# Attention steps of the next batch at other places in TensorE's order, first batch of four

## The reference

```python
# attention with decay: q, k, v, alpha are (4, 8, 768, 48)
for t in range(S):
    state = alpha[:, :, t, :, None] * state + einsum('bhd,bhe->bhde', k[:, :, t], v[:, :, t])
    y[:, :, t] = einsum('bhd,bhde->bhe', q[:, :, t], state)
x = y as (batch, seq, heads * head_dim)              # (4, 768, 384)
# first MLP: U (768, 32), V (32, 768), w_ch1 (384, 1536), w_ch2 (1536, 384)
h = x.transpose(0, 2, 1) @ U @ V
u = x + h.transpose(0, 2, 1)
x = u + maximum(u @ w_ch1, 0) @ w_ch2
# second MLP: w_in (384, 1024), w_spatial (768, 768), w_out (512, 384)
h = maximum(x @ w_in, 0); u, v = the two halves of h
v = (v - mean(v)) / sqrt(var(v) + 1e-6)
out = (u * (einsum('ts,bsd->btd', w_spatial, v) + b_spatial)) @ w_out
```

## Time and profile before

| | |
|---|---|
| median of 3 runs | 728.5 us (727.13 to 729.15) |
| the profiled execution | 727.21 us |
| its span, first to last instruction | 725.0 us |
| mean granted TensorE clock | 0.988 |
| TensorE busy | 696.3 us, 11336 matmuls |
| VectorE, ScalarE, GpSimd busy | 392.6, 340.2, 212.0 us |

### The profile page before, as it was taken

One profiled execution on the slowest core, in us unless ns is written; L12 is line 12 of the kernel. 1 busy time (PEld: TensorE's weight loads), 2 busy tenths in 40 slices (PEclk: granted clock), 3 DMA queues, 4 the chain that ended last, 5 costly groups with the idle time before them and its releaser, 6 DMA issues.

```text
span 725.0 us, 25711 instructions
## 1 busy us (share of the span) xinstructions
PE 696.3 (96%) x11336; PEld 660.6 (91%) x11336; DVE 392.6 (54%) x666; ACT 340.2 (47%) x575; POOL 212.0 (29%) x143
## 2 busy tenths in 40 slices
PE   2689999999999999999999999999999999999998
PEld 2688989899899999999999999999998998999998
DVE  6888665545654654655453415125834852871671
ACT  5887654554654454556444332335532432532422
POOL 6704660410450320351220330461360060043022
PEclk9879999999999999999999999999999999999999
DMA  9415410410401221401100341011110101101001
GB/s 360 169 47 168 163 42 8 154 47 10 149 3 46 80 79 46 156 3 47 37 3 3 101 151 66 33 38 62 65 45 23 66 23 43 65 0 65 0 0 65
DMA packets 16524, 49.48 MB, mean 68 GB/s; under 512 B 1616, under 2 KB 9552, under 8 KB 15920
## 3 DMA queue, kind: packets, MB, share of 16 engines
q1 hardware_dynamic: 16432, 48.09, 18.8%
HBM read 38.65 MB, written 9.44 MB: 66 GB/s over the span
## 4 chain that ended last, share of the span: by engine, by line
PE 92%; ACT 3%; DVE 2%; issue 1%; DMA 1%; SPq 0%; DVEq 0%; ACTq 0%
PE HB L906 25%; PE ZB L994 7%; PE ZB L996 7%; PE ZB L995 7%; PE SB L906 6%; PE SB L782 5%; PE SB L1031 5%; PE ZB L906 4%; PE SB L888 2%; PE SB L1035 2%; PE ZB L1031 2%; PE ZB L1044 2%; PE SB L897 2%; PE SB L843 2%; PE SB L1044 2%
## 5 line engine op out<-in xcount | busy, mean ns | idle before, releaser
L1556 DVE SCALAR_TENSOR_TENSOR hid_lo<-HB,hid_hi 128x384 fp32r<-128x384 f32 x92 | 51.2, 556 | 139.7 <-ACT hid_hi L1238 139.3
L1238 ACT ACTIVATE hid_hi<-HB 128x384 fp32r<-128x384 f32 x92 | 45.3, 492 | 158.6 <-PE HB L906 158.5
L994 PE MATMUL ZB<-hid_hi,w2h 128*128 128x384 f32 x288 | 98.2, 341 | 0.0
L906 PE MATMUL HB<-uh,w1h 128*128 128x384 f32 x276 | 97.8, 354 | 0.2 <-DVE ul L1552 0.2
L996 PE MATMUL ZB<-hid_lo,w2h 128*128 128x384 f32 x288 | 96.5, 335 | 0.0
L995 PE MATMUL ZB<-hid_hi,w2l 128*128 128x384 f32 x288 | 96.3, 334 | 0.0
L906 PE MATMUL HB<-ul,w1h 128*128 128x384 f32 x276 | 92.5, 335 | 0.0
L906 PE MATMUL HB<-uh,w1l 128*128 128x384 f32 x276 | 92.4, 335 | 0.1
L1085 ACT COPY Qd<-Q 48x768 f32<-48x768 f32 x84 | 73.1, 871 | 12.8 <-POOL Q L674 4.3
L731 POOL TENSOR_TENSOR gl<-gf,gh 128x384 fp32r<-128x384 f32 x32 | 33.5, 1048 | 144.1 <-ACT gh L1278 143.8
L674 POOL TENSOR_TENSOR Q<-Q,bk 112x768 f32<-112x768 f32 x14 | 25.6, 1827 | 162.7 <-ACT Qd L1085 162.7
(11 more groups left out here) (269 smaller groups left out, 1516.5 us busy)
## 6 DMA issues: line engine op xcount, KB each, us to landing
Q<-in_q SPq DMA_DIRECT2D x8, 768.0 KB, 6.1
AL<-in_al SPq DMA_DIRECT2D x7, 768.0 KB, 4.5
K<-in_k SPq DMA_DIRECT2D x7, 768.0 KB, 4.2
Vt<-in_v SPq DMA_DIRECT2D x8, 576.0 KB, 3.6
mid<-x2s SPq DMA_DIRECT2D x8, 576.0 KB, 3.7
x<-mid SPq DMA_DIRECT2D x4, 1152.0 KB, 5.4
out<-o_sb SPq DMA_DIRECT2D x24, 192.0 KB, 1.8
x2s<-in_w SPq DMA_DIRECT2D x9, 384.0 KB, 5.1
```

Source lines behind the costliest of these rows:

```text
L906: last = nc.tensor.matmul(dst, weights(x, w), moving(y, m), start=(n == 0 and x == y == 0), stop=(n == total - 1 and y == 1))
L994: nc.tensor.matmul(bank, w2h[:, i, cols], hi, start=(i == 0), stop=False)
L1238: nc.scalar.activation(hid_hi[:, i % HID, :], up_bank(i)[:, 0:TILE], ACT.Relu).then_inc(h_hi, 1)
L1556: nc.vector.scalar_tensor_tensor(hid_lo[:, i % HID, :], up_bank(i)[:, 0:TILE], 0.0, hid_hi[:, i % HID, :].bitcast(F32), ALU.max, ALU.subtr ...
```

## The change

For the first batch the places of the attention steps are no longer worked out by step_slots but written down, one unit index per step, group 0 and then group 1. The other batches keep step_slots.

```diff
 LEAD = [0.07] + [0.0] * (BATCH - 2)
-SLOTS = [step_slots(lead) for lead in LEAD]
+FIRST_SLOTS = [(8, 10, 12, 14, 16, 18, 20, 22, 24, 26, 26, 28, 28, 29), (31, 33, 35, 37, 39, 41, 43, 45, 47, 49, 49, 50, 50, 51)]
+SLOTS = [[[(g, n) for g in range(GROUPS) for n in range(STEPS) if FIRST_SLOTS[g][n] == j] for j in range(len(UNITS1))]]
+SLOTS += [step_slots(lead) for lead in LEAD[1:]]
```

## The result

| | before | after |
|---|---|---|
| median of 22 runs each | 726.93 us (724.74 to 730.2) | 725.49 us (723.81 to 727.42) |
| profiled execution, its span | 727.21, 725.0 | 724.95, 722.8 |

The ratio of the times is 0.9975, with a 95% interval of 0.9965 to 0.9985: by it 1.8 us were gained, between 1.1 and 2.5 (the two medians lie 1.44 apart). The forecast was a gain of 2.3 us, to 726.2.

What follows compares the result with a forecast made beforehand. TensorE was taken to bound the kernel, with holes in the first stretch to save. Gains of 1.5 + 0.77 = 2.3 us off a median of 728.5 gave 726.2 us, 0.32% faster; range 724.3 to 728.3.

Steps and rivals of the forecast that it cites:

- What bounds the kernel: Whole kernel: TensorE is 92% of the chain that ended last; the change moves only entries, so holes count.
- Level 5 and level 6: First stretch, group 0: level 5 behind h6, due 90.44; level 6 starts within 0.1 of 94.79, with h7 already done.
- The term "1.5": Group 0, ahead of level 6: one unit of 1.56 gained less 0.1, so 1.5 us, bounds 1.45 to 1.63.
- The term "0.77": Group 1, ahead of level 3: 2.43 in which h15 stood becomes 1.66, so 0.77 us gained.
- T to KV: Group 0: two units between instead of three; key copies hidden by 0.45, so 0, up to 0.5 us lost.
- AV and Y: Group 0: 0.13 should leave the AV pair and come to Y: 0, bounds 0.13 us either way.
- Levels 7 and T: Group 0: two holes of some 0.2 each stay: 0, bounds 0.45 us gained and 0.85 lost.
- Rival 3: Group 0: KV waits for ScalarE's key copies, 0.5 to 1.4 late; gain 1.8 to 0.9, 727.2 us; chance 0.11.
- Group 1: First stretch: level 3 goes behind h15, two units behind level 2, so the chain of 3.4 fits into 4.28; 0.77 gained.
- rival 1: VectorE let in earlier in group 0, between level 5's sums or before one at 6/7; 725.6 to 726.1; chance 0.13.
- Rivals 2 and 4: Group 0, levels 6 and 7: VectorE waits one more sum, 727.9, chance 0.14; or a whole GpSimd block, 730.0, chance 0.05.

Runs made afterwards that it cites:

- the run with group 0 alone: Against the changed kernel, group 1's steps got their old places back, so only group 0 has new ones; first stretch 115.12 us, profiled execution 724.77 us.

## Why the prediction was right, point by point

**What bounds the kernel.** Right. Nearly all of the gain lies in holes of TensorE in the first stretch. The other two stretches together take 226.6 to 227.0 before, and 227.0, 226.8 and 228.0 after.

**Level 5 and level 6.** The places came out as worked out: level 5 due at 90.44, measured 90.39; level 6 due at 94.72 or 0.15 late, measured 94.68, and 0.08 and 0.03 late in the next two profiles (the last against its own 4.31 per level). Both bounds for VectorE occurred: let in between the sums in the first profile (1.36), behind both in the other two (2.2), where the prediction had taken the second. The request came 2.02 behind the start of level 5 in every profile with the new place, not 1.68; it still fell into the first sum, so nothing hung on it. The cause was shown, not only argued: with the sums moved away the hole went in the old order of steps as well.

**What was mis-sized.** Three terms were, and they partly make up for each other, so it is partly luck that the sum of 2.3 came close to the 2.2 of the profiles.

The term "1.5" rests on a hole of 1.74 (0.12 + 1.62) in one profile. Against that profile it was right: from level 4 to KV 1.65 was gained, 0.03 of it ahead of level 7. But the hole has two sizes, 1.7 and 1.0. In the four profiles with the old places of group 0 and the sums where they were, level 4 to KV takes 23.64 in the mean, and in the four with the new places 22.38: 1.25 gained.

The term "0.77" of group 1 is 0.10 too large, and this in every profile. The unit of 2.43 did become 1.66. But T to KV was put at nothing, and the unit that goes from there stood between two units, where it costs 1.56; the unit that comes in ahead of level 3 has a step at its side and costs 1.66. From level 2 to KV it is 31.09 before (132.63 to 163.72) and 30.42 after (130.61 to 161.03), 0.67 gained:

```profile
163.72 1.10 PE L871 MATMUL SB<-Vt,bk 128*48 128x48 f32 x40
```

```profile
161.03 1.10 PE L873 MATMUL SB<-Vt,bk 128*48 128x48 f32 x40
```

(The unit of the earlier trace rows is itself one with a step at its side: it is h10, ahead of KV, and takes 1.65 from start to start. The 1.56 is right for z7 ahead of it, 106.93 to 108.49.)

The third term is that of AV and Y, below. Together the means give 1.25 + 0.67 + 0.2 = 2.1. The 44 timed runs say 1.8, between 1.1 and 2.5, so the two agree. Part of what is between them may be that the smaller hole is commoner than two in four; the runs that were timed have no profile, so that is open.

**Levels 7 and T.** Kept at 0: right, 0.21 and 0.24 over what the units take without the sums, before and after alike.

**T to KV.** The copies of the keys end at 106.36 + 1.22 = 107.58 and KV starts at 108.44, so the cover is 0.86, nearly twice the 0.45 of the prediction, because the end of the copies is 3.4 behind T and not 3.8. Rival 3 didn't happen.

```profile
104.15 0.49 ACT L1240 ACTIVATE hid_hi<-HB 128x384 fp32r<-128x384 f32 x1 [1.08 <-PE HB L908]
104.67 1.67 ACT L1138 COPY A<-Ad 32x768 f32<-32x768 f32 x2
106.36 1.22 ACT L1193 COPY bk<-SB 128x448 f32<-128x448 f32 x3
```

**AV and Y, group 0.** The units came as forecast: 1.65 now stands ahead of the AV pair (the second and third AV step, 128 matmuls), and 1.78 ahead of Y. What the prediction did not have is the pair itself. In the kernel before it took 1.81 from start to start and in the one after 1.50, and KV to Y fell from 8.80 to 8.48, where 0.13 either way was the bound:

```profile
113.78 1.88 PE L888 MATMUL SB<-Vt,A 128*32 128x48 f32 x128
115.59 0.45 PE L906 MATMUL HB<-uh,w1h 128*128 128x384 f32 x1
```

The pair took 1.7 or 1.8 in four of the six profiles with its old place and 1.50 in all six with the new one. Whether the place does that or chance is open: in group 1 the pair never moved, and it took between 1.63 and 2.07 in seven of the twelve.

**Group 1.** The mechanism was right: level 3's hole went in every profile with the new places and in none without. The size was 0.67, as worked out above.

**Rivals.** Half of rival 1 came true in one profile after of three and in the run with group 0 alone, at level 5 and not at 6 or 7, and was worth under 0.1. Rivals 2 and 4 needed longer scalings at levels 6 and 7; they took 3.21 to 3.23 in all orders that kept the sums. The chances split about evenly between more and less than 0.3%, and the measured 0.25% fell on the lower side; one outcome can't test them.

## What to carry to other kernels

A stall that the profile puts down to nothing may be an elementwise operation that ran late on a third engine: compare its duration with that of its twin one level earlier, and look at what GpSimd did meanwhile. Then either the consumer moves back or GpSimd's work moves to where VectorE has nothing urgent; the second takes away the cause and leaves no condition on the order (up to KV the old order then took 21.84 us and the new one 21.85). Before a hole of one profile goes into a sum, look at a second profile of the same kernel: here it was 1.7 us in two executions of the kernel before and 1.0 in the third. And a unit of work that moves away from two steps to a place between two units, or back, changes its own price: here by 0.1 us of 1.6.

## What the runs showed of the hardware

**VectorE can be passed over more than once.** The Trainium skill ("SBUF — State Buffer", Who interferes with whom) has the later of two such operations wait for the one in progress. Here VectorE, waiting since 90.57 while the weight piece was in progress, let two sums go by as well (until 93.88), and so it did in the second profile of before (4.04). In three other profiles in which it asked at the same place (3.10, 3.17 and 3.23) it got in ahead of the last sum. So the wait was not over with the operation in progress. At levels 6 and 7 it was passed over exactly once each time: it waited for the query scaling and for the first sum (3.23), while with no sum behind it took 2.26. In the second and third stretch, where one sum stands behind the query scaling, it was not passed over: 2.24 at 199.5, and the sum took 1.73.

**The outcome goes with an earlier meeting of the two.** In five profiles the weight piece beside level 4 started 0.13 to 0.23 behind that level, the key scaling of level 4 took 1.15 to 1.24, and GpSimd's query scaling behind it 1.94 to 2.02: the two had run into each other. In all five VectorE got in one operation earlier at level 5. In the five others with the sums in place the piece started 0.05 to 0.29 ahead of level 4 and the key scaling took 0.95 to 0.97; four of them had VectorE behind both sums, and one, the first profile after (0.97), between them. Why the earlier meeting should matter is open; no run was made for it.

**Small interruptions of TensorE move about.** The AV pair took 1.49 to 1.52 from start to start in 13 of 24 cases (two groups, twelve profiles), and up to 2.07 in the others. A unit took 0.3 longer between two matmuls of one product, where nothing is waited for: in the second stretch at the same place of the list in five of the twelve profiles, before (199.26 to 199.62) and after (196.67 to 197.01) among them. These interruptions are as large as the terms argued about here, and one reason why sums of single profiles came out 0.3 to 0.5 apart.
